# Retention scores computed per head on 64 rows, with scaling in halves and deeper load buffers

## The chip, the core and the metric

The kernel runs on one core of one Trainium2 chip. Five engines run their own instruction streams and meet at semaphores: TensorE (PE in the rows; its weight loads are shown apart as PEld), VectorE (DVE), ScalarE (ACT), GpSimd (POOL) and SyncE (SP), which here issues all the DMAs. The metric is the device time of one execution in microseconds.

## The reference

Three stages follow each other. The change touches the first alone, a decayed linear attention over 2 batches, 8 heads, 768 positions and 64 values a head:

```python
gamma = 1.0 - 2.0 ** (-5.0 - np.arange(H, dtype=np.float32))
for t in range(S):
    state = gamma[None, :, None, None] * state + np.einsum('bhd,bhe->bhde', k[:, :, t], v[:, :, t])
    y[:, :, t] = scale * np.einsum('bhd,bhde->bhe', q[:, :, t], state)
```

Then a layer norm and a two-layer MLP (`x + relu(norm(x) @ w_ch1) @ w_ch2`, 512 to 2048 to 512), then four attention experts of which each token takes the best two by a gate, with a softmax over causal scores and an output projection.

## The kernel before, in words

Retention is done in chunks. Two heads make a pair; 2 batches with 4 pairs give eight passes (`it` = 0 to 7), each over six chunks of 128 positions. The decay is put into k and q by two tables of factors (`decay_sb`), so that inside a chunk y is `(causal * (q k^T)) v`, and between chunks a running state `k^T v` carries the rest. One pass does, for its pair:

- VectorE multiplies the loaded k and q of the pass by their factors (`scale_rows`, L262): one instruction over 128 x 768 values for k and one for q.
- TensorE turns them, three chunks at a time (`turn`, L546), into two PSUM banks; ScalarE copies the result to `k_t` and `q_t` (`turned`, L897 and L901). `k_t` is padded: for each chunk it holds two 128 x 128 tiles, one per head, with the other head's 64 rows at zero. GpSimd writes these zeros once at the start (L433), and ScalarE fills a k unit by two copies of 64 rows.
- TensorE computes the scores of two chunks and two heads at a time (`chunk_scores`, L558): four matmuls with all 128 rows as contraction. The result is one PSUM bank, and two banks are used in turn. VectorE multiplies it by the causal mask into `prob` (`apply_causal`, L1126).
- `chunk_outputs` has the matmul of the state (`kv`, L571), the two of `prob` with v (L579) and the one of the state with q (L584). VectorE masks the state to its two heads (`state_out`, L1135), ScalarE copies y to `x` (L906).

An fp32 matmul that isn't a transpose stands in the trace as two weight loads and two matmul records, so four score matmuls are "x8".

The order is written out by hand. On TensorE a pass goes: scores 1, outputs 0, turn, outputs 1, turn, scores 2, outputs 2, turn, outputs 3, turn, outputs 4, scores 0 of the next pass, outputs 5, where the turns are for the next pass. On VectorE: mask 1, state 0, state 1, mask 2, state 2, state 3, state 4, mask 0 of the next pass, then the scaling of k and q for the pass after next (`scale_next`). In the last pass, steps of the first layer norm stand between these. SyncE issues k, q, v of each pass into two buffers in turn, each tensor as two DMAs, one a head, and after the last pass' loads the weights of the MLP; GpSimd splits these into two parts. The tiles of the MLP take the place of the retention's, so all of its work after the first hidden tiles waits for the last copy of y (`s_yx`).

At the start GpSimd writes identity matrices and masks; TensorE, ScalarE and VectorE all wait until its twelve constant instructions are done (`s_const`, 12), and VectorE also for a first ScalarE instruction (`s_preload`) that loads the table of the square root.

Of the kernel before, what the change touches and what calls it, by code (L numbers as in the profile page):

```python
# [69 lines left out]
def retention_moe_program(nc, q, k, v, g_ln, w_ch1, w_ch2, w_gate, wq, wk, wv, wo, out):  # L70
# [14 lines left out]
    AB = 3  # L85
    WIDE = (NC + 1) * P
# [3 lines left out]
    heads = {n: a.rearrange("b (i j) (c p) d -> (b i) j p c d", j=2, p=P) for n, a in (("q", q), ("k", k), ("v", v))}  # L90
# [9 lines left out]
    with ExitStack() as ctx:  # L100
# [53 lines left out]
        with ExitStack() as r:  # L154
            raw = {n: sb(r, f"raw_{n}", [P, 2, NC, 2, D]) for n in "qkv"}
            scaled = {n: sb(r, f"scaled_{n}", [P, 2, NC, 2 * D]) for n in "qk"}
# [42 lines left out]
        s_load = {n: [sem(f"s_load_{n}{m}") for m in range(2)] for n in "qkv"}  # L199
# [43 lines left out]
        T_STEPS = (2, 1, 2, 1)  # L243
        T_ALL = sum(T_STEPS)

# [3 lines left out]
        def s_bank(it, m_):  # L249
            return ps[:, 2 + (3 * it + m_) % 2, :].rearrange("p (c j t) -> p c j t", c=2, j=2)  # L250
# [7 lines left out]
        def scale_rows(engine, n, which):  # L258

            engine.wait_ge(s_load[which][n % 2], 32 * (n // 2 + 1))  # L260
            factors = decay[:, "qk".index(which), n, :].unsqueeze(2).broadcast_to((P, 2 * NC, D))
            engine.tensor_tensor(scaled[which][:, n % 2].rearrange("p c (j d) -> p (c j) d", j=2),  # L262
                                 raw[which][:, n % 2].rearrange("p c j d -> p (c j) d"), factors,
                                 ALU.mult).then_inc(s_scaled[which], 1)
# [91 lines left out]
        def _(sp):  # L356
            def load_heads(it):
# [42 lines left out]
            for it in range(NIT):  # L400
# [27 lines left out]
        def _(pool):  # L428
            pool.memset(ident[:, :], 0.0).then_inc(s_const, 1)
            pool.memset(ident_bf[:, :], 0.0).then_inc(s_const, 1)  # L430
            pool.memset(causal[:, :], 1.0).then_inc(s_const, 1)
            pool.memset(masked[:, :], 0.0).then_inc(s_const, 1)
            pool.memset(k_t[:, :, :, :, :], 0.0).then_inc(s_const, 1)  # L433
            pool.memset(same_head[:, :], 0.0).then_inc(s_const, 1)
            pool.wait_ge(s_const, 6)
            for j in range(2):
                pool.memset(same_head[j * D:(j + 1) * D, j * D:(j + 1) * D], 1.0).then_inc(s_const, 1)
            pool.wait_ge(s_const, 8)
            for m_ in (ident, ident_bf):
                pool.affine_select(out=m_[:, :], in_=m_[:, :], compare_op=ALU.not_equal, fill=1.0, base=0,  # L440
                                   pattern=[[-1, P]], channel_multiplier=1).then_inc(s_const, 1)

            pool.affine_select(out=causal[:, :], in_=causal[:, :], compare_op=ALU.is_ge, fill=0.0, base=0,
                               pattern=[[1, P]], channel_multiplier=-1).then_inc(s_const, 1)
            pool.affine_select(out=masked[:, :], in_=masked[:, :], compare_op=ALU.is_ge, fill=MASKED, base=0,
# [88 lines left out]
        def _(pe):  # L534

            def turn(n, unit):

                which, g = T_UNITS[unit]
                pe.wait_ge(s_scaled[which], n + 1)
                if unit >= 2:  # L540

                    pe.wait_ge(s_turned, T_ALL * n + sum(T_STEPS[:unit - 1]))
# [928 lines left out]
```

## Time and profile before

| | |
|---|---|
| median of three runs | 518.8 us (516.73 to 519.4) |
| the profiled execution | 520.72 us, of which the profile's span is 518.3 us |
| TensorE busy | 490.2 us (95%), weight loads 427.4 us |
| VectorE busy | 215.9 us (42%) |
| ScalarE busy | 160.9 us (31%) |
| GpSimd busy | 135.7 us (26%) |
| retention | from 0 to 95.8 us of the span |

The span holds the instructions of the core; the 2.4 us of the execution's time that are not in it lie around it. Busy times of TensorE are modelled at their ends. In the chain of waits the profile goes back from the last instruction to what released it, and "issue" there is time in which an engine waited for nothing that the profile shows.

### The profile page before, as it was taken

The page shows a single profiled execution, that of the slowest core. Times are in us where ns is not written, and L with a number is a line of the kernel's source. Part 1 is how long each engine was busy: PE and PEld are TensorE (multiplying, and loading weights), DVE is VectorE, ACT ScalarE, POOL GpSimd, SP SyncE. Part 2 cuts the span into 40 slices and gives each one's busy share as a digit, 9 for nine tenths or more (in the row PEclk, how much of TensorE's full clock was granted, in tenths as well). Part 3 has the DMA queues.
Part 4 walks back from the last instruction along what each step waited for, and adds up shares of the span by engine and source line. Part 5 has one row for each costly group of instructions (what it writes and reads, how often), then busy time and mean ns, then how long its engine had stood idle before and what let it go on. Part 6 is the DMA issues. An engine that isn't in the chain of part 4 may idle for free.

```text
span 518.3 us, 7613 instructions
## 1 busy us (share of the span) xinstructions
PE 490.2 (95%) x2784; PEld 427.4 (82%) x2784; DVE 215.9 (42%) x474; ACT 160.9 (31%) x370; POOL 135.7 (26%) x171
## 2 busy tenths in 40 slices
PE   3989989699999999999999999999999899999896
PEld 3989988588888888888888888888899799998775
DVE  2454464722243142221114111114445788878843
ACT  2333432210100122010012201004234567776732
POOL 3000001599993000000000000000220276755720
PEclk9999999899999999999999999999999999999999
DMA  9165453144460000000000000000025444443024
GB/s 220 32 148 126 93 119 106 49 135 141 129 178 22 0 1 0 0 0 0 0 0 0 0 1 0 1 0 1 5 48 131 103 103 118 100 99 93 2 82 162
DMA packets 65631, 33.04 MB, mean 64 GB/s; under 512 B 47296, under 2 KB 61760, under 8 KB 65600
## 3 DMA queue, kind: packets, MB, share of 16 engines
q1 hardware_dynamic: 65600, 32.63, 24.4%
q8 instruction: 19, 0.31, 0.2%
q14 instruction: 12, 0.10, 0.1%
HBM read 20.03 MB, written 3.15 MB: 45 GB/s over the span
## 4 chain that ended last, share of the span: by engine, by line
PE 81%; DVE 10%; issue 4%; ACT 3%; POOL 1%; DMA 0%; POOLq 0%; DVEq 0%; ACTq 0%
PE ps L638 26%; PE ps L647 25%; PE ps L742 5%; PE ps L558 4%; PE ps L797 3%; PE ps L714 3%; PE ps L579 2%; PE ps L762 2%; PE ps L780 2%; DVE neg_max L1351 2%; PE ps L824 2%; PE ps L571 2%; PE ps L546 2%; PE ps L584 2%; DVE scaled_k L262 1%
## 5 line engine op out<-in xcount | busy, mean ns | idle before, releaser
L1248 DVE SCALAR_TENSOR_TENSOR h_t_lo<-ps,h_t_hi 128x512 fp32r<-128x512 f32 x48 | 33.2, 691 | 195.2 <-ACT h_t_hi L947 195.2
L947 ACT ACTIVATE h_t_hi<-ps 128x512 fp32r<-128x512 f32 x48 | 28.7, 598 | 219.5 <-PE ps L638 219.5
L638 PE MATMUL ps<-xn_t_hi,w_hi 128*128 128x512 f32 x192 | 76.2, 397 | 1.1 <-DVE xn_t_lo L1243 1.1
L638 PE MATMUL ps<-xn_t_lo,w_hi 128*128 128x512 f32 x192 | 75.7, 394 | 0.0
L638 PE MATMUL ps<-xn_t_hi,w_lo 128*128 128x512 f32 x192 | 75.7, 394 | 0.0
L647 PE MATMUL ps<-w_hi,h_t_hi 128*128 128x512 f32 x192 | 75.2, 392 | 0.0
L647 PE MATMUL ps<-w_lo,h_t_hi 128*128 128x512 f32 x192 | 74.7, 389 | 0.0
L647 PE MATMUL ps<-w_hi,h_t_lo 128*128 128x512 f32 x192 | 74.7, 389 | 0.0
L475 POOL TENSOR_SCALAR raw_qk<-raw_qk 128x256 f32<-128x256 f32 x4 | 1.6, 409 | 211.1 <-PE ps L647 210.7
L504 POOL TENSOR_SCALAR a<-a,inv_den,weight 128x768 f32<-128x768 f32 (+5 forms) x48 | 34.1, 721 | 53.8 <-DVE inv_den L1371 53.5
L638 PEld LDWEIGHTS ps<-xn_t_hi,w_hi 128*128 128x128 f32 x192 | 36.7, 191 | 9.0 <-POOL w_lo L452 1.3
L638 PEld LDWEIGHTS ps<-xn_t_hi,w_lo 128*128 128x128 f32 x192 | 36.6, 191 | 7.8
L638 PEld LDWEIGHTS ps<-xn_t_lo,w_hi 128*128 128x128 f32 x192 | 36.8, 191 | 7.6
L647 PEld LDWEIGHTS ps<-w_hi,h_t_lo 128*128 128x128 f32 x192 | 36.0, 188 | 7.5
L647 PEld LDWEIGHTS ps<-w_hi,h_t_hi 128*128 128x128 f32 x192 | 36.0, 188 | 7.3
L647 PEld LDWEIGHTS ps<-w_lo,h_t_hi 128*128 128x128 f32 x192 | 36.1, 188 | 7.2
L1017 ACT ACTIVATE a<-ps,neg_max 128x768 f32<-128x768 f32 (+5 forms) x48 | 30.9, 645 | 19.3 <-DVE neg_max L1351 19.3
L450 POOL TENSOR_SCALAR w_hi<-raw_w 128x512 fp32r<-128x512 f32 x16 | 10.1, 632 | 74.3 <-DMA raw_w<-in_moe_w_ch 74.3
L558 PE MATMUL ps<-q_t,k_t 128*128 128x128 f32 x192 | 27.4, 289 | 1.8 <-ACT q_t L897 1.8
L1126 DVE TENSOR_TENSOR prob<-ps,causal 128x512 f32<-128x512 f32 x24 | 16.5, 689 | 27.4 <-PE ps L558 27.4
L1351 DVE TENSOR_REDUCE neg_max<-ps 128x1 f32<-128x768 f32 (+5 forms) x48 | 27.5, 613 | 0.2 <-PE ps L766 0.2
L579 PE MATMUL ps<-raw_v,prob 128*128 128x64 f32 x192 | 27.1, 265 | 0.0
(136 smaller groups left out, 935.7 us busy)
## 6 DMA issues: line engine op xcount, KB each, us to landing
raw_w<-in_moe_w_ch SPq DMA_DIRECT2D x32, 256.0 KB, 2.6
raw_k<-in_k SPq DMA_DIRECT2D x16, 192.0 KB, 3.2
raw_q<-in_q SPq DMA_DIRECT2D x16, 192.0 KB, 3.6
raw_v<-in_v SPq DMA_DIRECT2D x16, 192.0 KB, 3.1
k_twice_hi<-pj_hi SPq DMA_DIRECT2D x32, 96.0 KB, 2.2
k_twice_lo<-pj_lo SPq DMA_DIRECT2D x32, 96.0 KB, 2.2
out_y<-out_sb SPq DMA_DIRECT2D x12, 256.0 KB, 2.0
q_both<-pj_hi SPq DMA_DIRECT2D x16, 96.0 KB, 2.1
```

The source lines that it names most:

```text
L504: pool.tensor_scalar(a[:, g % AB, c0:c1], a[:, g % AB, c0:c1], inv_den[:, u:u + 1], weight[:, u, e:e + 1], ALU.mult, ALU.mult).then_inc(s_ ...
L558: mm = pe.matmul(s_bank(it, m_)[:, c, j], k_t[:, it % 2, 2 * m_ + c, j, :], q_t[:, it % 2, 2 * m_ + c, :], start=True, stop=True)
L579: mm = pe.matmul(y_bank(it, m_)[:, c % 2, j], prob[:, m_, c % 2, j, :], raw["v"][:, it % 2, c, j], start=(j == 0), stop=(c == 0), skip_gro ...
L638: mm = pe.matmul(ps[:, f % 2, :], w1[a_][:, f, kk, :], xn_t[b_][:, kk, :], start=(kk == 0 and p_ == 0), stop=(kk == KT - 1 and p_ == 2))
L647: mm = pe.matmul(ps[:, 2 + tau, :], h_t[a_][:, f % 2, tau * P:(tau + 1) * P], w2[b_][:, f, :], start=(f == 0 and p_ == 0), stop=(f == NF - ...
L714: mm = pe.matmul(v_bank(t), x2[a_][:, b, kk, c * P:(c + 1) * P], w_vg[b_][:, kk, :], start=(kk == 0 and p_ == 0), stop=(kk == KT - 1 and p ...
L742: mm = pe.matmul(pj_bank(n), w_qk[a_][n // 4 % 2][:, kk, :], x2[b_][:, b, kk, half_cols(n)], start=(kk == 0 and p_ == 0), stop=(kk == KT - ...
L947: act.activation(h_t["hi"][:, f % 2, :], ps[:, f % 2, :], ACT.Relu).then_inc(s_hhi, 1)
L1017: act.activation(a[:, g % AB, c0:c1], sc_bank(g, c1)[:, c0:c1], ACT.Exp, bias=neg_max[:, 2 * (g % 2) + w:2 * (g % 2) + w + 1], accum_out=d ...
L1126: dve.tensor_tensor(prob[:, m_].rearrange("p c j t -> p (c j) t"), s_bank(it, m_).rearrange("p c j t -> p (c j) t"), causal[:, :].unsqueez ...
L1248: dve.scalar_tensor_tensor(h_t["lo"][:, f % 2, :], ps[:, f % 2, :], 0.0, f32(h_t["hi"][:, f % 2, :]), ALU.max, ALU.subtract).then_inc(s_hl ...
L1351: top = dve.tensor_reduce(neg_max[:, 2 * (g % 2) + w:2 * (g % 2) + w + 1], sc_bank(g, c1)[:, c0:c1], AX.X, ALU.max, negate=True)
```

## The change

- `k_t` holds each chunk once, without zeros. The score matmul of a head takes the 64 rows of that head from `k_t` and `q_t`: rows 0 to 63 for the first, rows 64 to 127 for the second. The first head's scores of two chunks go to PSUM bank 2, the second's to bank 3. So both banks are one buffer, and scores wait for the mask of the scores before them, not of those before these.
- ScalarE fills a k unit by one copy of 128 rows.
- Scaling is done in halves of three chunks (128 x 384), and the four halves of a pass stand apart between the masks and states.
- q, k, v and the scaled tiles have three buffers; a tensor of a pass is one DMA, with the heads apart in the buffer. The first pass is loaded in pieces of three chunks, k and q first.
- GpSimd writes the constants in the order of their need, without the zeros; TensorE and ScalarE wait for the first two, VectorE's first mask for seven, and the rest is waited for behind the MLP.

```diff
-            k_t = sb(r, "k_t", [P, 2, NC, 2, P])
+            k_t = sb(r, "k_t", [P, 2, NC, P])
...
-        def s_bank(it, m_):
-            return ps[:, 2 + (3 * it + m_) % 2, :].rearrange("p (c j t) -> p c j t", c=2, j=2)
+        def s_bank():
+
+            return ps[:, 2:4, 0:2 * P].rearrange("p j (c t) -> p j c t", c=2)
...
+        def wait_loaded(engine, n, which, g):
+
+            if n == 0:
+                engine.wait_ge(s_first[which][g], 32)
+            else:
+                engine.wait_ge(s_load[which][n % RB], 16 * (n // RB + (n % RB > 0)))
+
+        def scale_rows(engine, n, which, g):
+
+            wait_loaded(engine, n, which, g)
+            factors = decay[:, "qk".index(which), n, 2 * G * g:2 * G * (g + 1)].rearrange("p (c j) -> p c j", j=2)
+            engine.tensor_tensor(scaled[which][:, n % RB, part_of(g)].rearrange("p c (j d) -> p c j d", j=2),
+                                 raw[which][:, n % RB, :, part_of(g)].rearrange("p j c d -> p c j d"),
+                                 factors.unsqueeze(3).broadcast_to((P, G, 2, D)),
                                  ALU.mult).then_inc(s_scaled[which], 1)
...
             def load_heads(it):
 
                 for n in "kqv":
-                    if it >= 2:
+                    if it >= RB:
                         if n == "v":
-                            sp.wait_ge(s_y, 3 * (it - 1))
+                            sp.wait_ge(s_y, 3 * (it - RB + 1))
                         else:
-                            sp.wait_ge(s_scaled[n], it - 1)
-                    for j in range(2):
-                        sp.dma_start(raw[n][:, it % 2, :, j, :], heads[n][it, j]).then_inc(s_load[n][it % 2], 16)
+                            sp.wait_ge(s_scaled[n], 2 * (it - RB + 1))
+                    sp.dma_start(raw[n][:, it % RB], heads[n][it]).then_inc(s_load[n][it % RB], 16)
...
             def chunk_scores(it, m_):
 
-                pe.wait_ge(s_turned, T_ALL * it + (3 if m_ == 0 else T_ALL))
-                if 3 * it + m_ >= 2:
-
-                    pe.wait_ge(s_prob, 3 * it + m_ - 1)
+                pe.wait_ge(s_turned, 4 * it + (2 if m_ == 0 else 4))
+                if 3 * it + m_ >= 1:
+
+                    pe.wait_ge(s_prob, 3 * it + m_)
                 for c in range(2):
                     for j in range(2):
-                        mm = pe.matmul(s_bank(it, m_)[:, c, j], k_t[:, it % 2, 2 * m_ + c, j, :],
-                                       q_t[:, it % 2, 2 * m_ + c, :], start=True, stop=True)
+                        rows = slice(j * D, (j + 1) * D)
+                        mm = pe.matmul(s_bank()[:, j, c], k_t[rows, it % 2, 2 * m_ + c, :],
+                                       q_t[rows, it % 2, 2 * m_ + c, :], start=True, stop=True)
...
-            def scale_next(n):
-
-                dve.wait_ge(s_kv, (NC - 1) * (n - 1))
-                scale_rows(dve, n, "k")
-                dve.wait_ge(s_t, 4 * (n - 1))
-                scale_rows(dve, n, "q")
+            def scale_next(n, which, g):
+
+                if n >= NIT:
+                    return
+                if n >= RB:
+                    dve.wait_ge(s_t, 4 * (n - RB) + 4)
+                    if which == "k":
+                        dve.wait_ge(s_kv, (NC - 1) * (n - RB + 1))
+                scale_rows(dve, n, which, g)
...
                 state_out(it, 0)
                 next_step(first)
+                scale_next(it + 2, "k", 0)
                 state_out(it, 1)
...
+                scale_next(it + 2, "q", 0)
                 for _ in range(3):
                     next_step(second)
                 state_out(it, 3)
+                scale_next(it + 2, "k", 1)
                 for _ in range(2):
                     next_step(first)
                 state_out(it, 4)
                 if it < NIT - 1:
                     apply_causal(it + 1, 0)
-                if it < NIT - 2:
-                    scale_next(it + 2)
+                scale_next(it + 2, "q", 1)
```

The instruction streams show what moves. The first place is VectorE's queue at the start, before:

```order
L262 TENSOR_TENSOR scaled_k<-raw_k,decay_sb 128x768 [waits s_tab,s_load_k0,s_const,s_preload]
L262 TENSOR_TENSOR scaled_q<-raw_q,decay_sb 128x768 [waits s_load_q0]
L1126 TENSOR_TENSOR prob<-ps,causal 128x512 [waits s_s]
L262 TENSOR_TENSOR scaled_k<-raw_k,decay_sb 128x768 [waits s_load_k1]
L262 TENSOR_TENSOR scaled_q<-raw_q,decay_sb 128x768 [waits s_load_q1]
L1126 TENSOR_TENSOR prob<-ps,causal 128x512 [waits s_s]
```

And the same place in the changed kernel, up to the second mask:

```order
L272 TENSOR_TENSOR scaled_k<-raw_k,decay_sb 128x384 [waits s_first_k0,s_tab]
L272 TENSOR_TENSOR scaled_q<-raw_q,decay_sb 128x384 [waits s_first_q0]
L272 TENSOR_TENSOR scaled_k<-raw_k,decay_sb 128x384 [waits s_first_k1]
L272 TENSOR_TENSOR scaled_q<-raw_q,decay_sb 128x384 [waits s_first_q1]
L1147 TENSOR_TENSOR prob<-ps,causal 128x2x2x128 [waits s_s,s_const,s_preload]
L272 TENSOR_TENSOR scaled_k<-raw_k,decay_sb 128x384 [waits s_load_k1]
L272 TENSOR_TENSOR scaled_q<-raw_q,decay_sb 128x384 [waits s_load_q1]
L272 TENSOR_TENSOR scaled_k<-raw_k,decay_sb 128x384 [waits s_load_k1]
L272 TENSOR_TENSOR scaled_q<-raw_q,decay_sb 128x384 [waits s_load_q1]
L1147 TENSOR_TENSOR prob<-ps,causal 128x2x2x128 [waits s_s]
```

The first scaling no longer waits for the constants and the preload, and its unit is a half; the mask waits for them in its place.

The second place is VectorE's queue around the end of a pass, here from mask 2 of pass 2 to state 1 of pass 3, before:

```order
L1126 TENSOR_TENSOR prob<-ps,causal 128x512 [waits s_y,s_s]
L1135 TENSOR_TENSOR state<-ps,same_head 128x128 [waits s_y,s_kv] x3
L1126 TENSOR_TENSOR prob<-ps,causal 128x512 [waits s_y,s_s]
L262 TENSOR_TENSOR scaled_k<-raw_k,decay_sb 128x768 [waits s_load_k0,s_kv]
L262 TENSOR_TENSOR scaled_q<-raw_q,decay_sb 128x768 [waits s_load_q0,s_t]
L1126 TENSOR_TENSOR prob<-ps,causal 128x512 [waits s_y,s_s]
L1135 TENSOR_TENSOR state<-ps,same_head 128x128 [waits s_y,s_kv] x2
```

The changed kernel at such a place, from mask 2 of pass 1 to state 1 of pass 2:

```order
L1147 TENSOR_TENSOR prob<-ps,causal 128x2x2x128 [waits s_y,s_s]
L1156 TENSOR_TENSOR state<-ps,same_head 128x128 [waits s_y,s_kv]
L272 TENSOR_TENSOR scaled_q<-raw_q,decay_sb 128x384 [waits s_load_q0,s_t]
L1156 TENSOR_TENSOR state<-ps,same_head 128x128 [waits s_y,s_kv]
L272 TENSOR_TENSOR scaled_k<-raw_k,decay_sb 128x384 [waits s_load_k0,s_kv,s_t]
L1156 TENSOR_TENSOR state<-ps,same_head 128x128 [waits s_y,s_kv]
L1147 TENSOR_TENSOR prob<-ps,causal 128x2x2x128 [waits s_y,s_s]
L272 TENSOR_TENSOR scaled_q<-raw_q,decay_sb 128x384 [waits s_load_q0,s_t]
L1147 TENSOR_TENSOR prob<-ps,causal 128x2x2x128 [waits s_y,s_s]
L1156 TENSOR_TENSOR state<-ps,same_head 128x128 [waits s_y,s_kv]
L272 TENSOR_TENSOR scaled_k<-raw_k,decay_sb 128x384 [waits s_load_k1,s_kv,s_t]
L1156 TENSOR_TENSOR state<-ps,same_head 128x128 [waits s_y,s_kv]
```

Between mask 0 and mask 1 of a pass there now stands one half in place of two whole scalings; the other three halves lie between states. TensorE's order of matmuls is the same in both kernels; only the value of `s_prob` that a score waits for has changed.

## Rows read from the trace of the kernel before

**Rows 1.** The stretches view; the columns are named in its first row.

```profile
core 0: us, PE busy (x) PEld busy (x) DVE busy (x) ACT busy (x) POOL busy (x), PEclk, DMA share, GB/s
3.00:4.00 1.00, 0.00 (x0) 0.00 (x0) 0.00 (x0) 0.00 (x0) 1.00 (x2) 1.00 1.22 274
99.50:106.50 7.00, 6.12 (x15) 4.85 (x16) 2.71 (x4) 2.20 (x4) 6.71 (x8) 0.53 0.48 137
106.50:110.00 3.50, 3.50 (x17) 2.83 (x16) 1.23 (x2) 0.60 (x1) 3.37 (x4) 1.00 0.52 151
```

**Rows 2.** The chain that ended last: start us, us, what.

```profile
27.54 0.46 PE ps L571 x2
...
33.31 0.91 PE ps L558 x8
...
34.84 0.95 DVE scaled_k L262
...
77.89 0.46 PE ps L571 x2
```

**Rows 3.** Timeline of the first 17 us: start us, us, engine, line, what.

```profile
1.19 1.08 SPq L366 DMA_DIRECT2D raw_k<-in_k  x2
...
1.35 2.67 POOL L433 MEMSET k_t<- 128x3072 f32 x1
...
5.87 0.21 ACT L933 ACTIVATE rvar<-ident 128x4 f32<-128x4 f32 x1 [3.79 <-POOL masked L445]
6.11 0.96 DVE L262 TENSOR_TENSOR scaled_k<-raw_k,decay_sb 128x768 f32<-128x768 f32 x1 [6.11 <-ACT rvar L933]
...
6.47 1.44 SPq L366 DMA_DIRECT2D raw_q<-in_q  x2
...
7.21 0.87 PE L546 MATMUL ps<-ident,scaled_k 128*128 128x128 f32 x3 [7.21 <-DVE scaled_k L262]
...
9.68 2.07 PE L558 MATMUL ps<-q_t,k_t 128*128 128x128 f32 x8 [0.79 <-ACT q_t L897]
...
13.99 2.07 PE L558 MATMUL ps<-q_t,k_t 128*128 128x128 f32 x8 [0.96 <-ACT q_t L897]
...
16.71 0.28 DVE L1135 TENSOR_TENSOR state<-ps,same_head 128x128 f32<-128x128 f32 x1
```

**Rows 4.** DMA issues of the first 110 us, with median us to landing.

```profile
raw_q<-in_q SPq DMA_DIRECT2D x16, 192.0 KB, 3.6
```

**Rows 5.** Timeline around the end of one pass, same columns as rows 3.

```profile
33.93 0.53 PEld L579 LDWEIGHTS ps<-raw_v,prob 128*128 128x128 f32 x4
34.24 0.69 DVE L1126 TENSOR_TENSOR prob<-ps,causal 128x512 f32<-128x512 f32 x1 [1.27 <-PE ps L558]
...
34.60 0.97 PEld L558 LDWEIGHTS ps<-q_t,k_t 128*128 128x128 f32 x8
34.71 1.06 PE L558 MATMUL ps<-q_t,k_t 128*128 128x128 f32 x8
...
36.58 0.68 DVE L1126 TENSOR_TENSOR prob<-ps,causal 128x512 f32<-128x512 f32 x1
...
37.18 0.28 DVE L1135 TENSOR_TENSOR state<-ps,same_head 128x128 f32<-128x128 f32 x1
37.58 0.30 PEld L571 LDWEIGHTS ps<-raw_v,scaled_k 128*128 128x128 f32 x2 [1.10 <-issue]
```

**Rows 6.** Groups by line and form, first 110 us: busy, mean ns, idle before.

```profile
L579 PEld LDWEIGHTS ps<-raw_v,prob 128*128 128x128 f32 x192 | 25.7, 195 | 0.0
L901 ACT ACTIVATE k_t<-ps 64x384 f32<-64x384 f32 x32 | 15.5, 485 | 29.0 <-PE ps L546 28.7
```

**Rows 7.** Timeline around the end of the seventh pass, as rows 3.

```profile
87.21 0.30 PEld L571 LDWEIGHTS ps<-raw_v,scaled_k 128*128 128x128 f32 x2 [0.62 <-issue]
```

**Rows 8.** Timeline from the last pass to the MLP, as rows 3.

```profile
95.43 0.38 ACT L906 ACTIVATE x<-ps 128x256 f32<-128x256 f32 x1 [1.68 <-PE ps L584]
...
100.38 0.77 PE L638 MATMUL ps<-xn_t_hi,w_hi 128*128 128x512 f32 x1 [1.14 <-DVE xn_t_lo L1243]
```

More of the change, by code:

```diff
@@ L154, in retention_moe_program @@
         with ExitStack() as r:
[L155 to L157 removed]
+            raw = {n: sb(r, f"raw_{n}", [P, RB, 2, NC, D]) for n in "qkv"}
+            scaled = {n: sb(r, f"scaled_{n}", [P, RB, NC, 2 * D]) for n in "qk"}
+            k_t = sb(r, "k_t", [P, 2, NC, P])
             q_t = sb(r, "q_t", [P, 2, NC, P])
@@ L198, in retention_moe_program @@
         s_wraw, s_gcol = sem("s_wraw"), sem("s_gcol")
-        s_load = {n: [sem(f"s_load_{n}{m}") for m in range(2)] for n in "qkv"}
+        s_first = {n: [sem(f"s_first_{n}{g}") for g in range(2)] for n in "qkv"}
+        s_load = {n: [sem(f"s_load_{n}{m}") for m in range(RB)] for n in "qkv"}
         s_scaled = {n: sem(f"s_scaled_{n}") for n in "qk"}
@@ L256, in kv_bank, with part_of @@
             return ps[:, 6 + it % 2, 0:P]
[L258 to L263, printed above, removed]
+        def part_of(g):
+            return slice(G * g, G * g + G)
+        def wait_loaded(engine, n, which, g):
[9 more added lines that the diff above has]
+                                 factors.unsqueeze(3).broadcast_to((P, G, 2, D)),
                                  ALU.mult).then_inc(s_scaled[which], 1)
@@ L399, in _ @@
             sp.dma_start(decay[:, :, :, :], tables[:, :, :, :]).then_inc(s_tab, 16)
-            for it in range(NIT):
+            for g in range(2):
+                for n in "kq":
+                    load_first(n, g)
+            for g in range(2):
+                load_first("v", g)
+            for it in range(1, NIT):
                 load_heads(it)
@@ L538, in turn @@
                 which, g = T_UNITS[unit]
-                pe.wait_ge(s_scaled[which], n + 1)
+                pe.wait_ge(s_scaled[which], 2 * n + g + 1)
                 if unit >= 2:
-                    pe.wait_ge(s_turned, T_ALL * n + sum(T_STEPS[:unit - 1]))
+                    pe.wait_ge(s_turned, 4 * n + unit - 1)
                 elif n >= 1:
-                    pe.wait_ge(s_turned, T_ALL * (n - 1) + sum(T_STEPS[:unit + 3]))
+                    pe.wait_ge(s_turned, 4 * (n - 1) + unit + 3)
                 for c in range(G):
-                    mm = pe.transpose(t_bank(unit)[:, c * P:(c + 1) * P], scaled[which][:, n % 2, G * g + c, :],
+                    mm = pe.transpose(t_bank(unit)[:, c * P:(c + 1) * P], scaled[which][:, n % RB, G * g + c, :],
                                       ident[:, :])
@@ L578, in chunk_outputs @@
                 for j in range(2):
-                    mm = pe.matmul(y_bank(it, m_)[:, c % 2, j], prob[:, m_, c % 2, j, :], raw["v"][:, it % 2, c, j],
+                    mm = pe.matmul(y_bank(it, m_)[:, c % 2, j], prob[:, m_, c % 2, j, :], raw["v"][:, it % RB, j, c],
                                    start=(j == 0), stop=(c == 0), skip_group_check=True)
@@ L894, in turned @@
                 chunks = slice(G * g, G * g + G)
-                src = t_bank(unit).rearrange("p (c t) -> p c t", c=G)
-                if which == "q":
-                    act.activation(q_t[:, n % 2, chunks, :], src, ACT.Copy).then_inc(s_turned, 1)
-                else:
-                    for j in range(2):
-                        rows = slice(j * D, (j + 1) * D)
-                        act.activation(k_t[rows, n % 2, chunks, j, :], src[rows], ACT.Copy).then_inc(s_turned, 1)
+                act.activation((q_t if which == "q" else k_t)[:, n % 2, chunks, :],
+                               t_bank(unit).rearrange("p (c t) -> p c t", c=G), ACT.Copy).then_inc(s_turned, 1)
             def y_out(it, m_):
@@ L1177, in retention @@
                     next_step(second)
+            dve.wait_ge(s_tab, 16)
+            for g in range(2):
+                for n in "kq":
+                    scale_rows(dve, 0, n, g)
             dve.wait_ge(s_preload, 1)
-            dve.wait_ge(s_const, 12)
-            dve.wait_ge(s_tab, 16)
-            scale_rows(dve, 0, "k")
-            scale_rows(dve, 0, "q")
+            dve.wait_ge(s_const, 7)
             apply_causal(0, 0)
-            scale_rows(dve, 1, "k")
-            scale_rows(dve, 1, "q")
+            for g in range(2):
+                for n in "kq":
+                    scale_rows(dve, 1, n, g)
             for it in range(NIT - 1):
```

49 lines of the change are left out of this document (28 added, 21 removed).

## The prediction, made before the changed kernel ran

> **What bounds the kernel now.** I read the table of busy times first: TensorE is busy 95% of the span, so whatever shortens its queue counts, and no other engine is near it. Then I asked where in the retention, the first 95.8 us, TensorE is not streaming. The chain of waits answers: one pass follows another every (77.89 - 27.54) / 5 = 10.07 us [rows 2], and in each the chain goes through TensorE except for one piece, where VectorE scales k and q and then masks. The timeline shows the price: the weight load of the next pass' second state matmul stands 1.10 us idle [rows 5]. All else in the pass is weight loads back to back: the six between 33.93 and 34.60 take 0.67 us, 0.11 us each, and this holds for the matmuls with 64 moving columns as for those with 128 [rows 5, 6]; the eight of a score group take 0.90 (0.91 in the chain, [rows 2]). 80 of them make 8.97 us, with the idle 1.10 the 10.07. So a pass is 80 weight loads and one wait for VectorE. DMA isn't a bound there. At the start it is another matter: nothing runs on VectorE until 6.11 us, since it waits for ScalarE, which waits for GpSimd's constants, 2.67 us of them the zeros of `k_t` [rows 3]; and the DMA engines move 274 GB/s, all they can [rows 1]. Every saving ahead of the last copy of y at 95.43 moves the MLP by as much, as everything there waits for it [rows 8].
>
> **The start.** Removed: the wait for constants and preload ahead of the first scaling, half of its length, and one of two ScalarE copies a k unit. The k of the first pass, 192 KB for its first half behind 96 KB of factors, is issued from 1.19 on; a full tensor lands at most 3.6 us after its issue [rows 4], so by 5.3; at 274 GB/s the missing half is 0.7 us earlier and queueing less, and I estimate 4.2. A half scaling costs, between 128 x 128 in 0.28 and 128 x 768 in 0.96 [rows 3, 5], by a straight line 0.55. Turns then begin at 4.2 + 0.1 + 0.55 + 0.14 (from the end of scaling at 7.07 to 7.21) = 5.0, 2.2 earlier. The single copy of 0.485 [rows 6] in place of two brings 0.25 in the first score group (TensorE's q turn ends only 0.2 before the second copy does) and 0.4 in the second. That is 2.85 us. What is late next is the load of pass 1: VectorE's queue now has four halves of pass 1 ahead of the second mask. Its raw q was issued at 6.47 as two DMAs, so the last lands by 7.2 + 3.6 = 10.8, three halves later it is 12.45; the mask now at 16.1 (0.6 before the state at 16.71, [rows 3]) can gain 3.6 at most. TensorE works at the lower pace here (eight loads in 2.07, [rows 3], not 0.90), and a later step to the higher pace could eat some. I take 2.9 without pairing of the scores and 3.4 with it, bounds 1.0 and 3.6. The three buffers, one DMA a tensor and the order of the last constants I cost at nothing: bytes stay the same, and the loads of a pass have a whole pass of 10 us to land in 3.6. With the cover gone (loads late by a microsecond at the start) the price is that microsecond, once.
>
> **Scaling in halves.** 4 x 0.55 = 2.2 us a pass in place of 1.9; VectorE has the room. Between mask 0 and mask 1 stands one half in place of both scalings. What is late next is TensorE, because of the single score buffer: scores 1 now wait for mask 0, which ends at 34.24 + 0.69 = 34.93; with the 0.12 from the end of a state (37.46) to the weight load (37.58) they begin at 35.05 and not at 34.60, 0.45 later [rows 5]. The half (34.93 to 35.5) lies beside them. They end at 34.71 + 1.06 + 0.45 = 36.22, mask 1 starts at 36.26, and as the weight load comes 1.00 after the start of mask 1 (36.58 to 37.58) it comes at 37.26, 0.32 earlier. Six passes have this scaling at their end: -1.9. The seventh has none (its idle is 0.62, [rows 7]) and only gets the wait, +0.45. Together -1.5. Queued behind the new wait are scores 1, outputs 0 and a turn, and VectorE's mask 1 waits for them; that is in the sum.
>
> **Scores on 64 rows.** Number and columns of the instructions stay: 24 loads a pass. No row shows a matmul on fewer than 128 rows, so I bound it. If two halves of the array don't work side by side: 0. If they do, load 2 of a head runs beside load 1 of the other; in the order (head 0, head 1, head 0, head 1), two loads each, eight take five slots, which saves 3 x 0.1125 = 0.34 a group. 24 groups less the two counted in the start are 22: 7.5 us. The saving passes through both places where VectorE is waited for, as masks start when scores end. A third possibility is a loss: the change from full to half array may cost something at each switch. In a pass three switches lie open on TensorE's path (into and out of scores 2, into scores 0; those around scores 1 and behind scores 0 lie beside waits), 23 in all. From below 0; from above a wait for the last matmul to end, which is 34.71 + 1.06 = 35.77 where the next load would follow at 34.60 + 0.90 = 35.50: 0.27 each, 6.2 us in all. No row is near either end, and I take the middle, 0.14 and 3.2 us. Side by side I hold for likelier than not, since the loads that set the pace go to different rows.
>
> The Trainium skill's "TensorEngine Tiling (Array Packing)", section "Key Properties", says that tiles can load weights and multiply in parallel, and that a change of tiling mode drains the engine. Taken whole, this would put the switch at its upper bound and the sum at -6.2, and it speaks against the change as much as for it; no row here shows either half.
>
> **Sum.** -3.4 - 1.5 - 7.5 + 3.2 = -9.2 us. Against the profiled execution, 520.72 (span 518.3 and 2.4 around it), that is 511.5; the median of the runs is 1.9 below that execution, so I forecast 518.8 - 9.2 = 509.6.
>
> **Rivals.**
> - No pairing, free switches: the half arrays take turns. For it speaks that one engine queue issues all loads and that 64 moving columns gain nothing over 128 today [rows 6]: the load alone sets the pace. -2.9 - 1.5 = -4.4, 514.4 us.
> - Slower: no pairing, and each of the 23 switches also lays bare the first load, 0.27 + 0.11 = 0.38, 8.7 us: -4.4 + 8.7 = +4.3, 523.1 us. From 0.19 a switch on the change costs time if there is no pairing. For it: 64-row tiles between 128-row ones six times a pass. Against: the 0.45 wait ahead of scores 1 hides part of it.
> - The MLP's first matmuls run at a granted clock of 0.53 for 7 us: 15 matmuls where the next 3.5 us hold 17 [rows 1], about 3.5 us lost, after TensorE had little to do between 95.4 and 100.38 [rows 8]. The gap stays, so I expect the loss again; but should the clock not fall there, with the forecast's other terms, 506.1. If on the contrary the start gains nothing because TensorE stays at the lower pace longer, 513.0.
> - The change of scores does pair with free switches: -12.4, 506.4 us.
>
> **How the numbers follow.** What a measurement of this kernel can tell from no change is about 0.5%, 2.6 us. Forecast and its neighbours with pairing (506 to 513): 0.50, of it a tenth below 506.4 or above 513. No pairing, free or cheap switches (513 to 516.2): 0.27. No pairing with switches of 0.1 to 0.3 us (516.2 to 521.4): 0.13. The slow rival: 0.10. So faster 0.78, same 0.12, slower 0.10. The range must reach the no-pairing case with some switch cost at the top and free pairing with part of the clock's loss gone at the bottom: 504.5 to 518.0. The forecast's own range is 506 to 513.
>
> **What would show it.** Score groups in the timeline of the new profile: weight loads of one group begun within 0.56 us (pairing) or 0.90 (none); a gap of 0.1 to 0.3 before and behind them for the switch. The idle in front of the second state matmul down from 1.10, the score group behind mask 0 waiting about 0.45. First scaling at 4.3, first turn at 5.0, the first state near 13.3. Passes of 8.7 us plus switches, against 9.75 without pairing. The last copy of y near 86. Wrong I'd be above all if the passes don't get shorter than 9.7, or if the loads of passes 0 to 2 hold VectorE beyond 12.5.

## The result, and the profile after

The changed kernel takes 511.66 us (median of four runs, 510.55 to 513.01), against 518.2 us before (four runs beside it, 516.73 to 519.4): a ratio of 0.9876, interval 0.9839 to 0.9913, or 6.5 us. The forecast was 509.6, or 9.2 us. The profiled execution took 511.56 us, with a span of 509.6; the span before was 518.3.

Where the 8.7 us of the two spans lie is found by laying the same event of both traces side by side. The weight load of the second state matmul of pass 1 is the first mark: 27.50 us before, 28.70 after, so the changed kernel is 1.2 us *behind* there. The timeline has the matmul itself, in the trace after, in passes 1 and 6:

```profile
28.73 0.46 PE L596 MATMUL ps<-raw_v,scaled_k 128*128 128x128 f32 x2
...
73.48 0.46 PE L596 MATMUL ps<-raw_v,scaled_k 128*128 128x128 f32 x2
```

That is (73.48 - 28.73) / 5 = 8.95 us a pass, where [rows 2] have 10.07: 5.6 us gained over five passes. The next mark is the MLP's start, then its second stage; the chain of waits has for after (start us, us, what)

```profile
94.93 5.74 PE ps L663 x24
100.67 2.72 PE ps L672 x12
```

and for before

```profile
100.38 8.42 PE ps L638 x24
108.80 1.36 PE ps L647 x6
```

So the MLP starts 5.45 us earlier, and its first 24 matmuls take 5.74 us and not 8.42. Ledger of this pair of profiles: start +1.2, five passes -5.6, seventh pass and layer norm -1.0, these 24 matmuls -2.7, all the rest -0.6: -8.7. What in it belongs to the kernels and what to these two executions, a second pair of profiles shows below.

Two of these entries are the clock of TensorE. At the MLP the fall to the lower of its two clock levels (1.2 and not 2.4 GHz), which [rows 1] show at 99.5 to 106.5 with a granted clock of 0.53, now lies ahead of the MLP's first matmul (third row), and is over when that starts. The other is at the start. The stretches view has, for after:

```profile
core 0: us, PE busy (x) PEld busy (x) DVE busy (x) ACT busy (x) POOL busy (x), PEclk, DMA share, GB/s
18.00:22.00 4.00, 4.00 (x22) 3.77 (x22) 1.45 (x3) 0.59 (x2) 0.00 (x0) 1.00 0.90 203
25.00:32.00 7.00, 6.98 (x65) 6.04 (x65) 3.92 (x9) 1.69 (x4) 0.00 (x0) 1.00 0.65 148
89.90:93.30 3.40, 3.40 (x18) 3.40 (x18) 2.38 (x7) 0.45 (x2) 1.69 (x2) 0.54 0.00 0
```

and for before:

```profile
18.00:22.00 4.00, 4.00 (x37) 3.94 (x37) 1.43 (x4) 2.38 (x6) 0.00 (x0) 1.00 0.00 0
```

Before, TensorE does 37 matmuls from 18 to 22 us; after, 22, which is the pace of the lower clock (the profile's clock column has 1.00 in either case, so here the counts have to be read). In the 4 us it loses (37 - 22) x 0.108 = 1.6 us. By the trace's clock records the higher level comes at 17.4 us before and at 24.8 after, so by an estimate from these counts it loses some 3 us in all.

The start itself, in the timeline after (start us, us, engine, line, what; compare [rows 3]):

```profile
3.99 0.56 DVE L272 TENSOR_TENSOR scaled_k<-raw_k,decay_sb 128x384 f32<-128x384 f32 x1 [3.99 <-DMA raw_k<-in_k]
...
4.66 0.50 PEld L570 LDWEIGHTS ps<-ident,scaled_k 128*128 128x128 f32 x3 [4.66 <-POOL masked L469]
...
7.51 0.56 DVE L272 TENSOR_TENSOR scaled_q<-raw_q,decay_sb 128x384 f32<-128x384 f32 x1 [0.71 <-DMA raw_q<-in_q]
7.58 0.49 SPq L380 DMA_DIRECT2D raw_k<-in_k  x1
...
12.94 0.56 DVE L272 TENSOR_TENSOR scaled_q<-raw_q,decay_sb 128x384 f32<-128x384 f32 x1 [0.84 <-DMA raw_q<-in_q]
...
14.35 0.68 DVE L1147 TENSOR_TENSOR prob<-ps,causal 128x512 f32<-128x512 f32 x1
14.95 0.28 DVE L1156 TENSOR_TENSOR state<-ps,same_head 128x128 f32<-128x128 f32 x1
```

The first scaling is at 3.99 and the first turn at 4.66, 2.1 and 2.5 us earlier than before. But then the loads are late: both halves of q wait for their pieces (the second, at 7.51, for 0.71 us), SyncE is done with the pieces only at 7.58, and raw q of pass 1 comes at 12.94. Two more halves stand between it and mask 1 (14.35), so the first state is at 14.95, 1.8 us earlier than before.

Nor are the DMA engines full in that time. From 3 to 10 us they move 183 GB/s (first row, the changed kernel), where they move 272 in first_whole, an experiment below that has three loads for the first pass and not twelve (second row), and 269 before:

```profile
3.00:10.00 7.00, 4.08 (x20) 3.08 (x20) 2.93 (x5) 1.20 (x3) 0.55 (x3) 1.00 0.80 183
```

```profile
3.00:10.00 7.00, 3.47 (x17) 2.48 (x18) 2.38 (x5) 0.98 (x2) 0.54 (x2) 1.00 1.20 272
```

A pass, where [rows 5] have it before:

```profile
44.33 0.30 PEld L609 LDWEIGHTS ps<-state,q_t 128*128 128x128 f32 x2
...
44.81 0.55 PEld L583 LDWEIGHTS ps<-q_t,k_t 64*128 64x128 f32 x8 [0.18 <-issue]
...
45.49 0.30 PEld L596 LDWEIGHTS ps<-raw_v,scaled_k 128*128 128x128 f32 x2
...
46.10 0.37 PEld L570 LDWEIGHTS ps<-ident,scaled_k 128*128 128x128 f32 x3
46.21 0.28 DVE L1156 TENSOR_TENSOR state<-ps,same_head 128x128 f32<-128x128 f32 x1
...
46.60 0.30 PEld L596 LDWEIGHTS ps<-raw_v,scaled_k 128*128 128x128 f32 x2
```

The idle ahead of the second state matmul is gone but for 0.17 (46.21 + 0.28 and the usual 0.12 for the way from VectorE make 46.61; the turn's loads end at 46.10 + 0.33 = 46.43). The score group is labelled 64*128, and its eight loads take 0.55 us where [rows 5] have 0.97. Yet from the state matmul's loads at 44.33 (two, 0.22) to the first score load is 0.48 - 0.22 = 0.26 without a load, and from the last score load to the next one there are 0.31 by the single records, where 0.11 is usual.

### The profile page after: what moved, and what is told of

Same layout as the page of the kernel before. It is cut to its first block, busy times and chain, and to the rows that moved or that the text cites. A ratio compares the mean times of both kernels' runs of the same rounds, so it can differ in the third digit from the quotient of the medians.

```text
span 509.6 us, 7606 instructions
## 1 busy us (share of the span) xinstructions
PE 490.6 (96%) x2784; PEld 422.9 (83%) x2784; DVE 214.4 (42%) x490; ACT 153.7 (30%) x354; POOL 133.9 (26%) x170
## 4 chain that ended last, share of the span: by engine, by line
PE 85%; DVE 7%; ACT 2%; issue 2%; DMA 1%; SPq 1%; POOL 1%; POOLq 0%; ACTq 0%; DVEq 0%
PE ps L663 26%; PE ps L672 26%; PE ps L768 5%; PE ps L604 4%; PE ps L823 3%; PE ps L583 3%; PE ps L740 3%; PE ps L596 3%; PE ps L788 2%; PE ps L609 2%; PE ps L806 2%; DVE neg_max L1379 2%; PE ps L850 2%; PE ps L570 2%; SPq L370 1%
## 5 line engine op out<-in xcount | busy, mean ns | idle before, releaser
L663 PE MATMUL ps<-xn_t_hi,w_hi 128*128 128x512 f32 x192 | 75.0, 390 | 1.1 <-DVE xn_t_lo L1271 1.1
L604 PE MATMUL ps<-raw_v,prob 128*128 128x64 f32 x192 | 29.5, 280 | 0.0
L604 PEld LDWEIGHTS ps<-raw_v,prob 128*128 128x128 f32 x192 | 27.6, 207 | 0.8
L806 PE MATMUL ps<-ident,a 128*128 128x128 f32 x168 | 23.6, 277 | 3.4 <-DVE a_low_lo L1387 2.2
```

Of the source, the lines that this page charges most:

```text
L604: mm = pe.matmul(y_bank(it, m_)[:, c % 2, j], prob[:, m_, c % 2, j, :], raw["v"][:, it % RB, j, c], start=(j == 0), stop=(c == 0), skip_gr ...
L663: mm = pe.matmul(ps[:, f % 2, :], w1[a_][:, f, kk, :], xn_t[b_][:, kk, :], start=(kk == 0 and p_ == 0), stop=(kk == KT - 1 and p_ == 2))
L806: mm = pe.transpose(flat(4, 6, s0 + P)[:, s0:s0 + P], a[:, g % AB, s0:s0 + P], ident[:, :])
```

## The experiments

All are the changed kernel with one thing altered, unless said. The edits are cut to the lines that matter; "..." stands for lines left out.

**Full-row scores (padded).** `k_t` padded again, 128 rows, two banks in turn, two ScalarE copies; the zeros are written behind the identity.

```diff
-                        mm = pe.matmul(s_bank()[:, j, c], k_t[rows, it % 2, 2 * m_ + c, :],
-                                       q_t[rows, it % 2, 2 * m_ + c, :], start=True, stop=True)
+                        mm = pe.matmul(s_bank(it, m_)[:, c, j], k_t[:, it % 2, 2 * m_ + c, j, :],
+                                       q_t[:, it % 2, 2 * m_ + c, :], start=True, stop=True)
...
```

> The changed kernel with the scores as before: k_t padded, 128 rows, two PSUM banks in turn, two ScalarE copies a k unit. Everything else stays changed. Theory A (the passes got shorter because VectorE's scaling left the chain; the 64-row scores save nearly nothing on TensorE, since 0.45 us saved by pairing is paid back by two switches of 0.20, and only shorten the chain from scores 1 to the state): passes of 9.2 to 9.35 us, against 8.95 changed and 10.07 before; time 2 to 3 us above the changed kernel. Theory B (the 64-row scores brought most): passes of 9.8 or more, time 6 us above the changed kernel.

Passes of 9.30 us, as theory A has it: of the 1.12 us that a pass lost, 0.77 came from the rest of the change and 0.35 from the scores, which here means the 64 rows together with the single score buffer and the single copy of k; no run takes these apart. The timeline shows where the 0.35 is, not in the loads but in what is left of the wait for VectorE:

```profile
42.24 0.37 PEld L574 LDWEIGHTS ps<-ident,scaled_k 128*128 128x128 f32 x3
...
42.94 0.30 PEld L599 LDWEIGHTS ps<-raw_v,scaled_k 128*128 128x128 f32 x2 [0.33 <-issue]
```

The turn's loads end at 42.24 + 0.33, the state's begins at 42.94: 0.37 of wait, against 0.17. Counted load by load over a whole pass, a score group from its first load to the next is 0.89 us here, and 0.20 + 0.645 = 0.845 in the changed kernel for scores 0 and 2, 0.94 for scores 1, which also wait for mask 0: 2.68 against 2.63 a pass. The other 0.3 is 0.20 less wait ahead of this state matmul and 0.09 ahead of the third.

The time didn't follow theory A: 511.47 us (511.19 to 511.87), ratio 0.9863 (0.9846 to 0.9879), as fast as the changed kernel though eight passes are 2.8 us longer. In this profile the clock hides it. From 18 to 22 us this kernel has

```profile
18.00:22.00 4.00, 4.00 (x38) 3.94 (x37) 2.08 (x7) 1.75 (x4) 0.00 (x0) 1.00 0.88 199
```

38 matmuls, and it is at the second state matmul of pass 1 at 24.3 us, 4.4 ahead of the changed kernel. Nor does its clock fall anywhere before the MLP. In its second profile (below) the lead is smaller: 25.3 us at that matmul, against 27.0 in the changed kernel's second.

**Scaling in one place (scaled_together).** Still in halves and 64-row scores, but all four between masks 0 and 1.

```diff
-                scale_next(it + 2, "k", 0)
...
-                scale_next(it + 2, "q", 0)
...
-                scale_next(it + 2, "k", 1)
...
-                scale_next(it + 2, "q", 1)
+                for g in range(2):
+                    for n in "kq":
+                        scale_next(it + 2, n, g)
```

> The changed kernel, with all four halves of a scaling between mask 0 and mask 1, as both were before. Theory A: mask 1 waits for four halves again, passes of 9.9 to 10.0 us, some 6 us above the changed kernel. Theory B: passes of 9.1 at most, 1 us above.

519.67 us over ten runs (515.84 to 521.53), ratio 1.0002 (0.9971 to 1.0032): the whole gain in time is gone. Passes are 9.83 us, a little under the 9.9 to 10.0 expected: 0.88 of the 1.12 us is back. In the profile the MLP starts at 100.85, 5.9 us later than in the changed kernel, as theory A has it; another 2.7 us is TensorE's clock, whose fall (99.8 to 106.7 us) here lies on the first 24 matmuls of the MLP and makes them 8.42 us long. The wait is back where it was:

```profile
46.56 0.55 DVE L272 TENSOR_TENSOR scaled_k<-raw_k,decay_sb 128x384 f32<-128x384 f32 x1
...
47.97 0.55 DVE L272 TENSOR_TENSOR scaled_q<-raw_q,decay_sb 128x384 f32<-128x384 f32 x1
...
48.43 0.68 DVE L1147 TENSOR_TENSOR prob<-ps,causal 128x512 f32<-128x512 f32 x1
...
49.43 0.30 PEld L596 LDWEIGHTS ps<-raw_v,scaled_k 128*128 128x128 f32 x2 [1.02 <-issue]
```

**Heads apart (heads_apart).** The loop over heads outside that over chunks.

```diff
-                for c in range(2):
-                    for j in range(2):
+                for j in range(2):
+                    for c in range(2):
                         rows = slice(j * D, (j + 1) * D)
```

> The changed kernel with the score matmuls of a group in the order head 0, head 0, head 1, head 1. If loads of the two halves run side by side only when they follow each other in the queue: a group from its first load to the next engine work takes 1.09 us and not 0.645, a pass about 10.2 to 10.3 and not 8.95, 9 to 10 us above the changed kernel. If the engine looks further ahead and pairs them anyway: 8.95 and no change. A halfway case (one pair in the middle of a group) gives 0.98 a group and passes of 9.9.

511.66 us, ratio 0.986 (0.9837 to 0.9883), passes of 8.98 us. The weight loads:

```profile
38.45 0.36 PEld L570 LDWEIGHTS ps<-ident,scaled_q 128*128 128x128 f32 x3
38.98 0.53 PEld L583 LDWEIGHTS ps<-q_t,k_t 64*128 64x128 f32 x8 [0.17 <-issue]
39.63 0.30 PEld L596 LDWEIGHTS ps<-raw_v,scaled_k 128*128 128x128 f32 x2
```

The group takes 0.65 as before. The records of the group have two loads 0.01 apart, then the next two 0.1 later, though the four loads of one head (two matmuls) stand first in the queue. If a pair is one load of each head, the engine doesn't take the loads in the queue's order only, but looks ahead past the loads of the first head and fills the free half. The records don't name the head, so this is the likely reading and not a shown one: that any two half-row loads are paired, of one head too, would look the same, and no run has scores of one head alone. Shown is that the order of the heads in the queue doesn't matter. My five slots out of eight rested on strict order; it is four.

**First pass loaded whole (first_whole).** Three DMAs in place of twelve.

```diff
-            for g in range(2):
-                for n in "kq":
-                    load_first(n, g)
-            for g in range(2):
-                load_first("v", g)
+            for n in "kqv":
+                sp.dma_start(raw[n][:, 0], heads[n][0]).then_inc(s_first[n][0], 16)
...
```

> The changed kernel, with q, k and v of the first pass loaded whole, three DMAs in place of twelve. Theory C (SyncE's issues of 0.49 us each hold the loads of pass 1 back): raw q of pass 1 is there at about 10.5 us in place of 12.9, the first state at 13 in place of 14.95, though the first scaling starts at 4.5 to 5.2 in place of 3.99; 1 to 2 us faster than the changed kernel, but the moment at which TensorE gets its higher clock moves between executions and may hide it in the time. Rival (the DMA engines' rate is the bound): raw q of pass 1 at 12.5 or later, no gain or a loss of 0.5 us.

```profile
4.36 1.31 SPq L380 DMA_DIRECT2D raw_k<-in_k  x1
...
11.03 0.56 DVE L272 TENSOR_TENSOR scaled_q<-raw_q,decay_sb 128x384 f32<-128x384 f32 x1 [0.20 <-DMA raw_q<-in_q]
...
12.85 0.69 DVE L1144 TENSOR_TENSOR prob<-ps,causal 128x512 f32<-128x512 f32 x1 [0.32 <-PE ps L580]
```

Theory C holds: k of pass 1 is issued at 4.36 and not at 7.58, its q is there at 11.03, mask 1 is at 12.85 and the first state at 13.6 (13 was expected), though the first scaling comes 0.9 later. The time is 510.31 us (507.64 to 513.04), ratio 0.9855 (0.9822 to 0.9889): 1.3 us less than the changed kernel, with intervals that overlap. In this execution the higher pace was there at 18 us:

```profile
18.00:22.00 4.00, 4.00 (x39) 3.76 (x38) 2.28 (x6) 1.31 (x3) 0.00 (x0) 1.00 0.29 66
```

**q's pieces from ScalarE's queue (two_queues).** One execution. SyncE issues the pieces of k and then those of v.

```diff
...
+            for g in range(2):
+                for j in range(2):
+                    act.dma_start(raw["q"][:, 0, j, part_of(g)], heads["q"][0][:, j, part_of(g)]).then_inc(s_first["q"][g], 16)
```

> The changed kernel, with the four pieces of q of the first pass issued by ScalarE and not SyncE. Theory C (0.5 us of SyncE an issue): four issues less, so raw k of pass 1 is issued at 5.5 in place of 7.6 and raw q of pass 1 is there at 11 and not 12.9; first state near 13.5. If the DMA engines bound it, 12.9 and 15 as now.

508.99 us once. The rows bear out theory C a second time, with the bytes and their pieces unchanged, and from 3 to 10 us the DMA engines move 261 GB/s and not 183:

```profile
5.46 0.49 SPq L380 DMA_DIRECT2D raw_k<-in_k  x1
...
10.93 0.56 DVE L272 TENSOR_TENSOR scaled_q<-raw_q,decay_sb 128x384 f32<-128x384 f32 x1 [0.40 <-DMA raw_q<-in_q]
...
13.26 0.29 DVE L1157 TENSOR_TENSOR state<-ps,same_head 128x128 f32<-128x128 f32 x1
```

**Late start (late_start).** Everything waits for the last constant, as before, with a memset as long as the zeros of `k_t` among them.

```diff
...
-            dve.wait_ge(s_tab, 16)
-            for g in range(2):
-                for n in "kq":
-                    scale_rows(dve, 0, n, g)
-            dve.wait_ge(s_preload, 1)
-            dve.wait_ge(s_const, 7)
+            dve.wait_ge(s_preload, 1)
+            dve.wait_ge(s_const, 11)
+            dve.wait_ge(s_tab, 16)
+            for g in range(2):
+                for n in "kq":
+                    scale_rows(dve, 0, n, g)
```

> The changed kernel, with TensorE, ScalarE and VectorE all waiting at the start for the last constant, and with a GpSimd memset of 128 x 3072 of a tile not yet in use among them (it stands for the zeros of k_t), so that the first scaling starts near 6.1 as before. Theory C (the start ends on the loads of pass 1): mask 1 still waits for raw q of pass 1, there at 12.9, and the first state stays at 14.9 to 15.3; time within 1 us of the changed kernel. Rival (the constants were the gain of the start): first state at 16.5 or later, 1.5 us slower or more.

```profile
6.35 0.56 DVE L273 TENSOR_TENSOR scaled_k<-raw_k,decay_sb 128x384 f32<-128x384 f32 x1 [6.35 <-ACT rvar L957]
...
12.84 0.56 DVE L273 TENSOR_TENSOR scaled_q<-raw_q,decay_sb 128x384 f32<-128x384 f32 x1 [1.10 <-DMA raw_q<-in_q]
...
14.85 0.28 DVE L1159 TENSOR_TENSOR state<-ps,same_head 128x128 f32<-128x128 f32 x1
```

The first scaling starts 2.4 us later than in the changed kernel and the first state 0.1 earlier. The new order of the constants is worth nothing as long as twelve pieces go through one queue. The time is 509.58 us (508.67 to 514.11), ratio 0.9865 (0.9809 to 0.9921). By the medians that is 2.1 us less than the changed kernel, where I expected at most 1 of difference, with ranges that overlap. Its pace from 18 to 22 us is the higher one:

```profile
18.00:22.00 4.00, 4.00 (x39) 3.76 (x38) 2.23 (x7) 1.31 (x3) 0.00 (x0) 1.00 0.89 202
```

**Three profiles more (after_again, before_again, padded_again).** No edit, to see what belongs to the execution.

> The changed kernel again, for a second profile. If the moment of the rise to the higher clock belongs to the execution and not to the kernel, it lies elsewhere than at 25.1 us, anywhere from 10 to 25; if the half-row matmuls delay it, it lies near 25 again, as in the two other executions with them that load in pieces.

> The kernel before again, for a second profile. The rise lay at 17.7 and the fall at 99.6 for 6.8 us. If they belong to the execution, both lie elsewhere; a pass stays 10.07 us.

> The changed kernel with full-row scores on a padded k_t, again, for a second profile. Its higher clock came at 10.7 us, that of the changed kernel at 25.1 and 21.7. If half-row matmuls keep the clock down for longer, it lies below 19 again; if it belongs to the execution, it can lie anywhere between 10 and 25. Passes of 9.3 us either way.

Passes stay at 8.95, 10.07 and 9.30 to 0.01 us. The pace from 18 to 22 us stays nearly the same, the changed kernel's (first row) and the padded one's (second):

```profile
18.00:22.00 4.00, 4.00 (x25) 3.78 (x24) 1.61 (x4) 0.69 (x2) 0.00 (x0) 1.00 0.90 205
```

```profile
18.00:22.00 4.00, 4.00 (x38) 3.94 (x37) 2.40 (x6) 1.75 (x4) 0.00 (x0) 1.00 0.87 197
```

Before has 38, where it had 37. The moment of the rise itself moves, though. By the clock records it lay at 24.8 us in the first profile of the changed kernel and at 21.5 in the second, with full rows at 10.4 and 16.5, and before at 17.4 and 17.7. (The moments of the clock named in three of the expectations, 25.1, 21.7, 17.7 and 10.7, are read 0.3 us too late.)

The fall ahead of the MLP moves too: it was past the start of the MLP before (99.3 to 106.1 us), and in the second profile it lies at 92.8 to 99.6, so the first 24 matmuls take the short time there as well. The second pair of profiles thus has another ledger: start -0.7 (the second state matmul's load of pass 1 at 27.64 before, 26.98 after), five passes -5.6, seventh pass and layer norm -0.6, the 24 matmuls 0, all the rest -0.6: -7.5, from spans of 516.3 and 508.8. The entry of the MLP is chance. That of the start is chance in part: somewhere between a loss of 1.2 and a gain of 0.7 us. The passes' -5.6 is the same in both.

**Full rows and whole loads (padded_whole).** The two edits above together.

> Full-row scores on a padded k_t, and q, k, v of the first pass loaded whole. By the passes alone (9.30 against 8.95) it is 8 x 0.35 = 2.8 us slower than the changed kernel with whole loads (510.3). If half-row matmuls hold the clock down at the start, some of this comes back and it lies within 1 us of it.

511.64 us (510.78 to 511.9), ratio 0.9871 (0.984 to 0.9901). Passes of 9.30, and 1.3 us above the half rows with whole loads, between my two cases.

**Scores 0 and 1 as one group (merged_moved).** Four chunks and two heads in sixteen loads, from pass 1 on; the second half of q is scaled behind state 0.

```diff
...
+            def two_scores(it):
+                pe.wait_ge(s_turned, 4 * it + 4)
+                pe.wait_ge(s_prob, 3 * it)
+                for c in range(4):
+                    for j in range(2):
+                        rows = slice(j * D, (j + 1) * D)
+                        mm = pe.matmul(s_bank(c // 2)[:, j, c % 2], k_t[rows, it % 2, c, :],
+                                       q_t[rows, it % 2, c, :], start=True, stop=True)
+                mm.then_inc(s_s, 2)
...
-                    chunk_scores(it + 1, 0)
+                    two_scores(it + 1)
...
```

> The changed kernel, with scores 0 and 1 of a pass as one group of sixteen loads (scores 1 in the free halves of the same two banks), so that there are four switches a pass and not six; the second half of q is scaled behind state 0 and no longer between the masks. If a switch costs TensorE 0.20 us each: passes of 8.45 to 8.55 us, 3 us faster than the changed kernel. If the 0.20 is only the wait for the semaphore and not the switch: 8.9, within 0.5 us of it.

506.63 us (506.19 to 508.3), ratio 0.9761 (0.9714 to 0.9808), 5.0 us below the changed kernel where I expected 3; passes of 8.40, under the 8.45 to 8.55 expected. The weight loads:

```profile
40.73 0.30 PEld L619 LDWEIGHTS ps<-state,q_t 128*128 128x128 f32 x2
41.15 0.97 PEld L593 LDWEIGHTS ps<-q_t,k_t 64*128 64x128 f32 x16
42.24 0.52 PEld L614 LDWEIGHTS ps<-raw_v,prob 128*128 128x128 f32 x4
```

Sixteen loads go from 41.15 to 42.24, 1.09 us: the second eight cost 0.45. Ahead of them stands the same 0.20 (40.73 + 0.22 to 41.15), and the 1.09 are 0.89 for sixteen loads side by side and 0.20 behind them. One pair of switches less and no wait for mask 0 is 0.46 of the 0.55 that a pass loses. By the load records the rest is 0.03 in the loads of scores 1 and 0.06 in the wait ahead of the second state matmul.

**Both (best).** merged_moved with the first pass loaded whole.

> The same, with q, k, v of the first pass loaded whole, by three DMAs. Both gains should add: passes of 8.45 to 8.55, the first state at 13.9 as with whole loads alone; 4 to 5 us below the changed kernel. Rival: TensorE's clock rises late and the gain of the start is not seen in the time; then as merged_moved.

505.69 us (503.56 to 508.26), ratio 0.972 (0.9664 to 0.9776) to the kernel before: faster than both kernels, and all four runs lie below all four of the changed one. Passes of 8.40, the first state at 13.6. Over merged_moved it gains 0.9 us by the medians, within what the runs scatter. In the profiles the MLP starts at 88.00 and not at 90.06, but in this one, which is of the slowest of the four runs, the fall of the clock (82.6 to 92.9 us) reaches into its first 24 matmuls, which take 7.99 us and not 5.74.

## Why the prediction was right, and where it was off

**The bound and the place.** That a pass is 80 weight loads and one wait for VectorE held: scaled_together brings the wait back, and 0.88 of the 1.12 us a pass with it.

**Scaling in halves.** The half costs 0.55 as worked out:

```profile
L272 DVE TENSOR_TENSOR scaled_q<-raw_q,decay_sb 128x384 f32<-128x384 f32 x16 | 8.8, 551 | 2.6 <-DMA raw_q<-in_q 2.6
```

The term was mis-sized: I had 0.32 us a pass, and padded, with full rows and two score buffers, shows 0.77. The wait behind mask 0 that I priced at 0.45 is 0.06 beyond the switches: the switch out of scores 0 and that into scores 1 lie in the time in which mask 0 is made, 0.20 each. I had said that they lie beside the wait, and had still charged the wait in full. In the changed kernel, scores included, measured is -0.97 us a pass from the wait ahead of the second state matmul (1.14 to 0.17, counted from load to load; [rows 5] have the first as 1.10) and -0.09 at the third state matmul, a wait that I hadn't seen.

**Scores on 64 rows.** Here two terms were mis-sized against each other. I took 0.34 a group for the pairing and 0.14 a switch, 7.5 and 3.2 us. The runs give 0.45 a group (eight more loads in merged_moved take 1.09 - 0.645 = 0.45 in place of 0.89) and 0.20 a switch (merged_moved and the load records of all groups). Into and out of a group that is 0.40 against 0.45: on TensorE's path the half rows save 0.05 us a group. I had 0.60 us a pass from the scores and padded shows 0.35; 0.29 of it is time that TensorE no longer waits for masks and states. The Trainium skill's "TensorEngine Tiling (Array Packing)", "Key Properties", has both rules, parallel loads and a drain at a change of mode; by them the trace agrees, with 0.45 and 0.20 us. Its sum would have been -6.2 with my 0.27 for the drain.

The errors of the two parts cancelled for the most: by parts I had 9.15 us a pass (10.07 - 0.32 - 1.02 + 0.42) and measured was 8.95.

**The start.** This step failed. I forecast 3.4 us, and named the loads of pass 1 as what is late next, but with 10.8 us as their time, since "bytes stay the same". The number of issues doesn't: twelve of about 0.5 us, each with half the bytes of one of the old six, put the issue of k of pass 1 at 7.58 in place of 5.07, and its q is there only at 12.94. That the DMA engines move "all they can" I had read from one microsecond at 274 GB/s; with twelve small pieces in one queue they moved 183 GB/s from 3 to 10 us. The state came 1.8 us earlier and not 3.4. By late_start none of this is due to the constants. "With the cover gone the price is that microsecond" was right in kind; I had not counted the issues.

**The clock at the start.** I had this as part of a rival, "the start gains nothing because TensorE stays at the lower pace longer", 513.0 us. In kind that rival came true beside the forecast's own mechanism: the start was to gain 3.4 us, and one pair of profiles has a loss of 1.2, the other a gain of 0.7. The measured 511.66 lies between the two. The fourteen profiles fall into groups by the trace's clock records:

| profiles | scores | wait ahead of pass 0's second state matmul, us | higher clock from, us |
|---|---|---|---|
| after, after_again, heads_apart, scaled_together, merged_moved | half rows | 1.5 to 2.2, at the lower pace | 21.5 to 24.8 |
| first_whole, two_queues, late_start, best | half rows | none | 15.9 to 17.8 |
| before, before_again, padded_again, padded_whole | full rows | none | 16.5 to 17.7 |
| padded | full rows | 1.6, at the higher pace | 10.4 |

Half rows alone don't bring the late rise, as the second group has them too. What the five late ones share is that wait, at 15 to 16 us, with the clock still low. That it delays the rise is a likely reading, not a shown one: no run put the wait in by itself, and whether the half rows have a part in it stays open, as no full-row kernel waited there at the lower pace.

**The MLP's clock.** I had expected the loss there again, 3.5 us, and priced its absence as a rival. It was absent in both profiles of the changed kernel, and in the second one of the kernel before as well; in the first pair it accounts for 2.7 of the 8.7 us in the spans, in the second for nothing.

**The sum.** That 9.2 us were forecast and 6.5 measured is in part luck. The start gave 2.7 us less than forecast in the better pair of profiles. Against that stand 0.20 us a pass more than forecast, and 0.6 us behind the MLP's first 24 matmuls, which no term had and no run followed.

## What to carry to other kernels

Where an engine that is busy 95% still has one regular wait, look at what the engine it waits for does just before, and spread that: it gave more here than halving the array's rows (0.77 against 0.35 us a pass). Small tiles side by side pay on TensorE only if the groups are long: a change to them and back took 0.40 us here, and eight loads gained 0.45. Cutting first loads into pieces buys an earlier start and pays for it in the issuing queue, where the loads of the next stage stand; count issues as well as bytes.

## What the runs showed of the hardware that I had not expected

- Eight weight loads of half the rows, four of each head, take the time of four (0.45 us against 0.89 for eight of all rows). It makes no difference whether the heads alternate in the queue: with the two matmuls of one head first, the group took 0.65, otherwise 0.645.
- A change between 128-row and 64-row matmuls left 0.20 us without a weight load, in each direction, at the higher pace, and 0.35 at the lower.
- A DMA issue on SyncE didn't take longer for more bytes: 0.5 us for each piece of 96 KB in the changed kernel, and 0.50 for the first load of 384 KB in first_whole. The next ones of 384 KB there took 0.84, 1.69 and 1.31 us. With the twelve pieces in one queue the DMA engines moved 183 GB/s from 3 to 10 us, with four of them in a second queue 261, with three whole loads 272.
- An earlier start can go with a later rise of TensorE's clock: it came at 17.4 and 17.7 us in two executions of the kernel before, at 24.8 and 21.5 in two of the changed one. It also moves between executions of one kernel, by 6 us with full rows (10.4 and 16.5).
